# Attention ahead of two gated MLPs: each head's scores and values as matmuls on their own part of the TensorE array

## The chip, the cores and the metric

The kernel runs on one core of one Trainium2 chip. The metric is device time in microseconds from the first to the last instruction of one execution. The shown time of the kernel before is the median of three runs; the profile is one more execution, recorded by the hardware profiler.

## The reference

Shapes: q, k, v are (2, 8, 768, 64); the output is (2, 768, 512). All inputs are float32.

```python
# attention: a band of +-15 keys, and one key for each block of 32 (max of k, mean of v)
k_sum = k.reshape(B, H, nb, 32, D).max(axis=3)
v_sum = v.reshape(B, H, nb, 32, D).mean(axis=3)
scores_l = np.where(|i - j| < 16, scale * q @ k.T, -1e9)
scores_s = scale * q @ k_sum.T + log(32)
a = softmax(concat[scores_l, scores_s])
x = (a @ concat[v, v_sum])            # -> (B, S, H * D)
# first gated MLP: a causal depthwise convolution with 5 taps makes the gate
x = sigmoid(conv(x, conv_w)) * (x @ w_val) @ w_out
# second: gating through a matmul over the sequence
h = relu(x @ w_in); u, v = split(h)
v_n = layernorm(v)
out = (u * (w_spatial @ v_n + b)) @ w_out2
```

## The kernel before

**Stages.** The attention stage takes 54 steps and fills the first third of the execution. Behind it come `x @ w_val` with the convolution, the product of `w_out` and `w_in` ("fused"), the `u` and `v` products, the product with `w_spatial` and the output product. Those behind the attention are written as split fp32r matmuls, all in `product` (L858).

**Tiling of the attention.** The 16 (batch, head) pairs are taken two heads at a time: 8 pairs p of heads, six tiles t of 128 rows each, so 48 steps i. The two heads of a pair lie in partitions 0 to 63 and 64 to 127 (their 64 channels each). A tile of 128 rows is two groups of 64 rows; a group sees 96 near keys and 24 block keys, 120 in all.

- `turn_k`, `turn_q` (L739): TensorE transposes of k and q into PSUM, two for a piece of 256 rows; three pieces of k and three of q for each pair of heads, one piece a step. k of all 128 partitions is copied to `k_win` in one piece (VectorE, L1340).
- q is copied to `qT` in two pieces. `qT` is a block-diagonal array: for each group 128 columns, of which the first 64 hold head 0 in partitions 0 to 63 (ScalarE, L1022) and the last 64 hold head 1 in partitions 64 to 127 (VectorE, L1351). The other two quarters are zeros, written once at the start (L1401).
- `scores` (L774): one matmul for each of the two groups, with the 128x128 block of `qT` as the stationary operand and 128x120 of `k_win` moving. The zeros keep the heads apart: out come 64 rows of head 0 and 64 of head 1.
- `mask_scores` (VectorE, L1313), `exponentials` (ScalarE, L1034, two a step), `normalise` (VectorE, L1333).
- `turn_probs` (L788): two TensorE transposes a step; `take_probsT` (ScalarE, L1048) copies both out of PSUM.
- `values` (L803): one matmul for each group, 120x128 of `v_win` (both heads' channels) stationary and 120x128 of `probsT` (both heads' rows) moving. All four combinations of head and head come out; only the two diagonal blocks of 64x64 are used.
- `take_x` copies the attention output to `xT` once for every two steps: head 0's blocks on ScalarE (L1054), head 1's on ScalarE as well (L1057), or on VectorE (L1358) for the 7 of 24 that `x_on_dve` names.
- `means` (L815) sums v over blocks, three matmuls for each pair of heads.

**What sets the order.** Everything is written out by hand: each engine has its own loop over the steps and waits on semaphores. TensorE's step i is: scores(i), one turned piece of the next pair, turn_probs(i-5), values(i-6). ScalarE's is: take_probsT(i-5), turned_q, exponentials(i), take_x on even steps. SyncE issues all loads in one queue, two pairs ahead for k and q, one for v.

## Time and profile before

| | |
|---|---|
| median of 3 runs | 296.59 us (296.08 to 296.78) |
| the profiled execution | 294.5 us, of which 292.8 us are the span of the trace |
| granted TensorE clock | 1.00 (2.4 GHz) over the whole span |
| TensorE matmul busy | 282.2 us, 96%, 1828 matmuls |
| VectorE busy | 226.1 us, 77% |
| ScalarE busy | 181.4 us, 62% |
| GpSimd busy | 91.7 us, 31% |
| DMA engines, q1 | 35.0% of 16 engines' span |

The stages follow each other, so these shares are averages over stages with different limits. Matmuls are pipelined: one that is busy for 0.27 us lets the next one start 0.11 us later, so what a stretch of TensorE costs is read from starts, not from busy time. An fp32 matmul that is written once shows as two records, a transpose as one.

### The profile page before, as it was taken

To read this page: it belongs to the slowest core of one execution; us is meant where nothing else is said; L and a number is where in the kernel's file an instruction comes from. 1 tells how busy PE (TensorE), PEld (TensorE's weight loads), DVE (VectorE), ACT (ScalarE), POOL (GpSimd) and SP (SyncE) were. 2 spreads that over 40 slices of the span, in tenths; PEclk is the share of its full clock that TensorE was granted. 3 is DMA by queue.
4 is the path that set the end of the run, shared out by engine and by line. 5 is a ranking of instruction groups with operands and counts; after the bars stand their busy time and mean duration, and the time that the engine had idled before them with its cause. 6 is when DMAs were issued, how large, how long until landed. Compare 5 with 4: busy or idle time off the path is not lost.

```text
span 292.8 us, 5673 instructions
## 1 busy us (share of the span) xinstructions
PE 282.2 (96%) x1828; PEld 264.8 (90%) x1828; DVE 226.1 (77%) x632; ACT 181.4 (62%) x517; POOL 91.7 (31%) x111
## 2 busy tenths in 40 slices
PE   7879999999999999899999999999999999999996
PEld 7769999999989998798899988998889999999996
DVE  6798999999788989993202676895867989898952
ACT  3579999999998567454354455625258342644632
POOL 6425778898433898325000000000007000000000
PEclk9999999999999999999999999999999999999999
DMA  7998999999520443000040000000021000001324
GB/s 159 218 264 175 247 196 231 221 184 216 150 73 2 158 120 119 0 0 3 0 154 10 0 0 2 0 0 2 0 72 73 2 1 0 2 0 56 140 77 161
DMA packets 52474, 25.54 MB, mean 87 GB/s; under 512 B 44618, under 2 KB 48222, under 8 KB 52446
## 3 DMA queue, kind: packets, MB, share of 16 engines
q1 hardware_dynamic: 52446, 25.18, 35.0%
q8 instruction: 15, 0.25, 0.4%
q14 instruction: 13, 0.11, 0.1%
HBM read 22.03 MB, written 3.15 MB: 86 GB/s over the span
## 4 chain that ended last, share of the span: by engine, by line
PE 67%; ACT 17%; DVE 7%; issue 5%; POOL 2%; DMA 1%; DVEq 0%; ACTq 0%; POOLq 0%
PE psum L858 57%; ACT probs L1034 8%; DVE psum L1387 4%; PE psum L774 2%; ACT qT L1022 2%; PE psum L803 2%; ACT xT L1054 2%; PE psum L739 2%; PE psum L834 1%; ACT probsT L1048 1%; PE psum L788 1%; PE psum L935 1%; ACT xT L1057 1%; DMA raw<-in_moe_w_in_dram 1%; DVE work L1452 1%
## 5 line engine op out<-in xcount | busy, mean ns | idle before, releaser
L1034 ACT ACTIVATE probs<-neg_s,neg_max 128x120 f32<-128x120 f32 x96 | 36.8, 387 | 0.3 <-DVE neg_max L1313 0.3
L686 POOL TENSOR_TENSOR vn_lo<-vn_all,vn_hi 128x768 fp32r<-128x768 f32 x3 | 5.8, 1958 | 83.0 <-ACT vn_hi L1155 83.0
L803 PE MATMUL psum<-probsT,v_win 120*128 120x128 f32 x192 | 29.9, 278 | 0.0
L774 PE MATMUL psum<-k_win,qT 128*128 128x120 f32 x192 | 29.0, 274 | 0.7 <-DVE qT L1351 0.7
L1387 DVE SCALAR_TENSOR_TENSOR psum<-xT,conv_c,psum 128x384 f32<-128x384 f32 x48 | 26.0, 615 | 1.2 <-ACT psum L1076 1.2
L1313 DVE CUSTOM_DVE_ANT_0 neg_s<-psum,mask 128x120 f32<-128x120 f32 x96 | 24.5, 276 | 2.6 <-PE psum L774 2.2
L774 PEld LDWEIGHTS psum<-k_win,qT 128*128 128x128 f32 x192 | 25.2, 192 | 1.2 <-issue 0.9
L803 PEld LDWEIGHTS psum<-probsT,v_win 120*128 120x128 f32 x192 | 25.2, 191 | 0.4
L788 PE MATMUL psum<-ident,probs 128*120 128x128 f32 x96 | 19.1, 281 | 2.8 <-ACT probsT L1048 2.2
L1048 ACT ACTIVATE probsT<-psum 120x256 f32<-120x256 f32 x48 | 18.1, 376 | 3.4 <-PE psum L788 3.0
L1333 DVE TENSOR_TENSOR probs<-probs,psum 128x240 f32<-128x240 f32 x48 | 19.0, 400 | 1.0
L686 POOL TENSOR_TENSOR g_lo<-work,g_hi 128x384 fp32r<-128x384 f32 x16 | 15.9, 1019 | 11.8 <-ACT g_hi L1124 11.8
L1034 ACT ACTIVATION_READ_ACCUMULATOR probs<-neg_s,neg_max 128x1 f32 x96 | 18.6, 194 | 0.0
L788 PEld LDWEIGHTS psum<-ident,probs 128*120 128x120 f32 x96 | 11.1, 137 | 6.6 <-ACT probsT L1048 5.7
L1198 ACT ACTIVATE u<-psum 128x384 f32<-128x384 f32 x16 | 7.8, 487 | 14.0 <-PE psum L858 13.7
L1469 DVE TENSOR_TENSOR wsp_lo<-wsp_all,wsp_hi 128x1152 fp32r<-128x1152 f32 x3 | 4.0, 1355 | 14.5 <-ACT wsp_hi L1142 14.5
L686 POOL TENSOR_TENSOR x_lo<-xT,x_hi 128x768 fp32r<-128x768 f32 x8 | 14.6, 1829 | 0.6
L667 POOL COPY v_win<-v_mean 24x1536 f32<-24x1536 f32 x8 | 11.7, 1462 | 8.6 <-ACT v_mean L1064 7.5
L858 PE MATMUL psum<-g_hi,wu_hi 128*128 128x384 f32 x64 | 14.4, 346 | 0.0
L1076 ACT ACTIVATE psum<-xT,conv_c 128x384 f32<-128x384 f32 x16 | 8.7, 573 | 9.1 <-DVE gate L1387 9.1
L1526 DVE BATCH_NORM_STATS2 stats<-work 128x6 f32<-128x512 f32 x12 | 8.3, 691 | 7.7 <-ACT work L1209 7.7
L858 PE MATMUL psum<-x_hi,wval_hi 128*128 128x384 f32 x64 | 14.1, 341 | 0.0
(183 smaller groups left out, 829.4 us busy)
## 6 DMA issues: line engine op xcount, KB each, us to landing
v_win<-in_v_dram SPq DMA_DIRECT2D x16, 240.0 KB, 3.8
k_nat<-in_k_dram SPq DMA_DIRECT2D x16, 192.0 KB, 4.9
v_nat<-in_v_dram SPq DMA_DIRECT2D x8, 384.0 KB, 3.8
q_nat<-in_q_dram SPq DMA_DIRECT2D x14, 192.0 KB, 4.4
raw<-in_moe_w_spatial_dram SPq DMA_DIRECT2D x6, 384.0 KB, 3.1
raw<-in_moe_w_in_dram SPq DMA_DIRECT2D x8, 256.0 KB, 3.1
out_dram<-rows SPq DMA_DIRECT2D x12, 128.0 KB, 1.7
out_dram<-rows SPq DMA_DIRECT2D x6, 256.0 KB, 2.0
```

Source lines behind the costliest of these rows:

```text
L667: nc.gpsimd.tensor_copy(v_win[NEAR:KEYS, p % 2, :, :], src).then_inc(means_spread, 1)
L686: nc.gpsimd.tensor_tensor(dst_lo, src, dst_hi.bitcast(F32), ALU.subtract).then_inc(lo_sem, 1)
L774: ins = nc.tensor.matmul(bank_s(i)[:, g, :], qT[:, s, 2 * t + g, :], k_win[:, s, 2 * t + g, :], start=True, stop=True)
L788: ins = nc.tensor.transpose(bank_t[:, g, :], probs[:, i % RING, g, :], ident[:, :])
L803: ins = nc.tensor.matmul(bank_x(i)[:, i % 2 * 2 + g, :], v_win[0:KEYS, s, 2 * t + g, :], probsT[0:KEYS, i % 2, g, :], start=True, stop=True)
L858: ins = nc.tensor.matmul(o, lhs[a][c], rhs[b][c], start=(fresh and part == 0 and c == 0), stop=(part == 2 and c == n - 1), skip_group_chec ...
L1034: ins = nc.scalar.activation(probs[:, i % RING, g, :], neg_s[:, i % 3, g, :], ACT.Exp, bias=neg_max[:, i % 4, g:g + 1], scale=-1.0, accum_ ...
L1048: nc.scalar.activation(probsT[0:KEYS, i % 2, :, :], bank_t, ACT.Copy).then_inc(probsT_ready, 1)
L1076: nc.scalar.activation(psum[:, 4 + half, 0:HALF], x_of(p, half * HALF, HALF), ACT.Copy, scale=conv_c[:, (TAPS - 1) * C + c:(TAPS - 1) * C ...
L1313: nc.vector.tensor_tensor_reduce(out=neg_s[:, i % 3, g, :], in0=bank_s(i)[:, g, :], in1=mask[:, e, :], scale=-(float(D) ** -0.5), scalar=B ...
L1333: nc.vector.tensor_tensor(a, a, r, ALU.mult).then_inc(probs_ready, 1)
L1387: nc.vector.scalar_tensor_tensor(out=o, in0=x, scalar=w, in1=acc, op0=ALU.mult, op1=ALU.add).then_inc(conv_step, 1)
```

## The change

`scores` and `values` are cut by head. For each group and each head h there is one matmul of its own, on partitions and columns of its head alone:

- scores: stationary 64x64 of `qT` (64 channels of head h, 64 rows), moving 64x120 of `k_win`, output to PSUM partitions 64h to 64h+63. Head 0 uses rows 0 to 63 and columns 0 to 63 of the array, head 1 rows 64 to 127 and columns 64 to 127.
- values: stationary 120x64 of `v_win` (the head's channels), moving 120x64 of `probsT` (the head's rows), output to PSUM partitions 64h to 64h+63.

`qT` has 64 columns for each group in place of 128 and no zeros; its two memsets go. One ScalarE copy of 128x256 takes a piece of q; VectorE's is gone. `bank_x` has 64 columns for each group, and one ScalarE copy of 128x256 takes two steps' output; ScalarE's second copy and VectorE's seven are gone, and so is `x_on_dve`. Three semaphores stand where there were six.

```diff
-            qT = sb("qT", [P, 2, GROUPS, P], F32, att)
+            qT = sb("qT", [P, 2, GROUPS, GROUP], F32, att)
...
         def bank_x(i):
-            return psum[:, 6 + (i // 2) % 2, :].rearrange("p (g n) -> p g n", n=P)
-
-        def x_on_dve(j):
-            return j % 3 == 1 and 2 * j < STEPS - 4
+            return psum[:, 6 + (i // 2) % 2, 0:2 * P].rearrange("p (g n) -> p g n", n=GROUP)
...
             def scores(i):
...
                 if t % 2 == 0:
-                    pe.wait_ge(qA_ready, PIECES * p + t // 2 + 1)
-                    pe.wait_ge(qB_ready, PIECES * p + t // 2 + 1)
+                    pe.wait_ge(qT_ready, PIECES * p + t // 2 + 1)
...
                 for g in range(2):
-                    ins = nc.tensor.matmul(bank_s(i)[:, g, :], qT[:, s, 2 * t + g, :], k_win[:, s, 2 * t + g, :],
-                                           start=True, stop=True)
+                    for h in range(2):
+                        d, rows_of = slice(h * D, (h + 1) * D), slice(h * GROUP, (h + 1) * GROUP)
+                        ins = nc.tensor.matmul(bank_s(i)[rows_of, g, :], qT[d, s, 2 * t + g, :],
+                                               k_win[d, s, 2 * t + g, :], start=True, stop=True, skip_group_check=True)
...
             def values(i):
...
                 for g in range(2):
-                    ins = nc.tensor.matmul(bank_x(i)[:, i % 2 * 2 + g, :], v_win[0:KEYS, s, 2 * t + g, :],
-                                           probsT[0:KEYS, i % 2, g, :], start=True, stop=True)
+                    for h in range(2):
+                        d, rows_of = slice(h * D, (h + 1) * D), slice(h * GROUP, (h + 1) * GROUP)
+                        ins = nc.tensor.matmul(bank_x(i)[d, i % 2 * 2 + g, :], v_win[0:KEYS, s, 2 * t + g, d],
+                                               probsT[0:KEYS, i % 2, g, rows_of], start=True, stop=True,
+                                               skip_group_check=True)
...
         def _(act):
             def turned_q(p, piece):
...
-                nc.scalar.activation(qT[0:D, p % 2, n * piece:n * (piece + 1), 0:GROUP],
-                                     by_group(bank_qk(PIECES + piece)[0:D]), ACT.Copy).then_inc(qA_ready, 1)
+                nc.scalar.activation(qT[:, p % 2, n * piece:n * (piece + 1), :],
+                                     by_group(bank_qk(PIECES + piece)), ACT.Copy).then_inc(qT_ready, 1)
...
             def take_x(j):
...
-                nc.scalar.activation(by_group(x_of(p, r * P, 2 * P)[0:D]), bank_x(2 * j)[0:D, :, 0:GROUP],
-                                     ACT.Copy).then_inc(xA_ready, 1)
-                if not x_on_dve(j):
-                    nc.scalar.activation(by_group(x_of(p, r * P, 2 * P)[D:P]), bank_x(2 * j)[D:P, :, GROUP:P],
-                                         ACT.Copy).then_inc(xB_ready, 1)
+                nc.scalar.activation(by_group(x_of(p, r * P, 2 * P)), bank_x(2 * j), ACT.Copy).then_inc(x_ready, 1)
...
         def _(dve):
...
-            def turned_q(p, piece):
...
-            def take_x(j):
...
-            for s in range(2):
-                nc.vector.memset(qT[:, s, :, :], 0.0).then_inc(q_zeros, 1)
```

TensorE in the middle of the attention stage, a step and the start of the next, before. The numbers are output partitions x moving columns, and x2 counts matmuls as written (each fp32 matmul of L774 and L803 is two records in the trace):

```order
L739 MATMUL psum<-ident,k_nat 128x128 x2
L788 MATMUL psum<-ident,probs 120x128 x2
L803 MATMUL psum<-probsT,v_win 128x128 x2
L774 MATMUL psum<-k_win,qT 128x120 x2
L739 MATMUL psum<-ident,k_nat 128x128 x2
```

The same place after; the lines have other numbers there (L727, L775, L792, L761):

```order
L727 MATMUL psum<-ident,k_nat 128x128 x2
L775 MATMUL psum<-ident,probs 120x128 x2
L792 MATMUL psum<-probsT,v_win 64x64 x4
L761 MATMUL psum<-k_win,qT 64x120 x4
L727 MATMUL psum<-ident,k_nat 128x128 x2
```

The order of the kinds is the same. Values and scores are four matmuls each in place of two, and they alone don't use the whole array.

ScalarE over three steps in the middle of the stage, before:

```order
L1054 ACTIVATE xT<-psum 64x256
L1057 ACTIVATE xT<-psum 64x256
L1048 ACTIVATE probsT<-psum 120x256
L1022 ACTIVATE qT<-psum 64x4x64
L1034 ACTIVATE probs,sums<-neg_s,neg_max 128x120 x2
L1048 ACTIVATE probsT<-psum 120x256
L1022 ACTIVATE qT<-psum 64x4x64
L1034 ACTIVATE probs,sums<-neg_s,neg_max 128x120 x2
L1054 ACTIVATE xT<-psum 64x256
```

And after:

```order
L1040 ACTIVATE xT<-psum 128x256
L1034 ACTIVATE probsT<-psum 120x256
L1008 ACTIVATE qT<-psum 128x256
L1020 ACTIVATE probs,sums<-neg_s,neg_max 128x120 x2
L1034 ACTIVATE probsT<-psum 120x256
L1008 ACTIVATE qT<-psum 128x256
L1020 ACTIVATE probs,sums<-neg_s,neg_max 128x120 x2
L1040 ACTIVATE xT<-psum 128x256
```

The second copy of the attention output is gone, and the copies of q and of the output write 128 partitions in place of 64.

## Rows read from the trace of the kernel before

**Rows 1.** The page: busy time, share of the span, instructions of each engine.

```profile
PE 282.2 (96%) x1828; PEld 264.8 (90%) x1828; DVE 226.1 (77%) x632; ACT 181.4 (62%) x517; POOL 91.7 (31%) x111
```

**Rows 2.** Busy time by stretch; the last three columns: clock, DMA share, GB/s.

```profile
core 0: us, PE busy (x) PEld busy (x) DVE busy (x) ACT busy (x) POOL busy (x), PEclk, DMA share, GB/s
...
49.50:58.80 9.30, 9.09 (x79) 8.60 (x79) 8.98 (x48) 9.15 (x40) 7.88 (x10) 1.00 0.92 210
...
120.00:162.00 42.00, 42.00 (x231) 38.52 (x231) 19.12 (x33) 20.00 (x40) 7.96 (x8) 1.00 0.09 29
```

**Rows 3.** Chain that ended last, parts in the middle of the attention stage.

```profile
52.55 0.75 ACT probs L1034 x4
...
53.33 0.13 issue
53.47 0.37 ACT qT L1022
53.83 0.76 ACT probs L1034 x4
54.59 0.23 ACT xT L1054
```

**Rows 4.** ScalarE in order of time: start, length, line, operation.

```profile
51.11 0.36 ACT L1054 ACTIVATE xT<-psum 64x256 f32<-64x256 f32 x1
51.50 0.38 ACT L1057 ACTIVATE xT<-psum 64x256 f32<-64x256 f32 x1
51.90 0.38 ACT L1048 ACTIVATE probsT<-psum 120x256 f32<-120x256 f32 x1
```

**Rows 5.** TensorE in order of time, one step and the next.

```profile
49.49 0.43 PE L788 MATMUL psum<-ident,probs 128*120 128x128 f32 x2 [0.17 <-ACT probsT L1048]
49.76 0.62 PE L803 MATMUL psum<-probsT,v_win 120*128 120x128 f32 x4
50.22 0.60 PE L774 MATMUL psum<-k_win,qT 128*128 128x120 f32 x4
50.66 0.38 PE L739 MATMUL psum<-ident,q_nat 128*128 128x128 f32 x2
50.88 0.38 PE L788 MATMUL psum<-ident,probs 128*120 128x128 f32 x2
51.10 0.61 PE L803 MATMUL psum<-probsT,v_win 120*128 120x128 f32 x4
51.54 0.60 PE L774 MATMUL psum<-k_win,qT 128*128 128x120 f32 x4
```

**Rows 6.** TensorE in order of time: block means, then first values of four pairs.

```profile
53.73 0.82 PE L815 MATMUL psum<-v_nat,sel 128*120 128x128 f32 x6
54.38 0.38 PE L788 MATMUL psum<-ident,probs 128*120 128x128 f32 x2
...
18.11 0.61 PE L803 MATMUL psum<-probsT,v_win 120*128 120x128 f32 x4
...
46.66 0.68 PE L803 MATMUL psum<-probsT,v_win 120*128 120x128 f32 x4
55.92 0.67 PE L803 MATMUL psum<-probsT,v_win 120*128 120x128 f32 x4
...
84.82 0.68 PE L803 MATMUL psum<-probsT,v_win 120*128 120x128 f32 x4
```

**Rows 7.** The page's groups: busy us, mean ns of one.

```profile
L774 PE MATMUL psum<-k_win,qT 128*128 128x120 f32 x192 | 29.0, 274 | 0.7 <-DVE qT L1351 0.7
```

**Rows 8.** TensorE later: matmuls of 384 columns, then of 256.

```profile
102.40 0.85 PE L858 MATMUL psum<-x_hi,wval_hi 128*128 128x384 f32 x4
103.09 0.85 PE L858 MATMUL psum<-x_hi,wval_lo 128*128 128x384 f32 x4
...
262.39 0.40 PE L858 MATMUL psum<-wout_hi,g_hi 128*128 128x256 f32 x2
262.62 0.40 PE L858 MATMUL psum<-wout_hi,g_lo 128*128 128x256 f32 x2
```

**Rows 9.** TensorE in the last six steps of the attention.

```profile
87.42 0.38 PE L788 MATMUL psum<-ident,probs 128*120 128x128 f32 x2
87.64 0.61 PE L803 MATMUL psum<-probsT,v_win 120*128 120x128 f32 x4
88.00 0.96 PE L858 MATMUL psum<-x_hi,wval_hi 128*128 128x384 f32 x4
88.80 0.38 PE L788 MATMUL psum<-ident,probs 128*120 128x128 f32 x2
```

**Rows 10.** ScalarE and VectorE groups by form; last, one line's durations min/median/max.

```profile
L1048 ACT ACTIVATE probsT<-psum 120x256 f32<-120x256 f32 x48 | 18.1, 376 | 3.4 <-PE psum L788 3.0
L1022 ACT ACTIVATE qT<-psum 64x256 f32<-64x256 f32 x24 | 8.8, 371 | 2.6 <-PE psum L739 2.4
...
L1351 DVE COPY qT<-psum 64x256 f32<-64x256 f32 x24 | 10.2, 427 | 1.0 <-PE psum L739 0.3
...
L1057 ACT ACTIVATE xT<-psum x17: 378/378/382, 23.6 to 93.0; 64x256 f32<-64x256 f32 x17
```

**Rows 11.** Chain that ended last, at the start of the attention stage.

```profile
15.71 0.43 DVE qT L1351
...
17.08 0.44 DVE qT L1351
```

**Rows 12.** SyncE's queue in order of time; then v's small loads, last number us to landing.

```profile
44.70 3.00 SPq L520 DMA_DIRECT2D k_nat<-in_k_dram  x2
...
51.97 0.42 SPq L534 DMA_DIRECT2D v_win<-in_v_dram  x1
...
54.61 1.74 SPq L520 DMA_DIRECT2D k_nat<-in_k_dram  x2
...
v_win<-in_v_dram SPq DMA_DIRECT2D x32, 20.0 KB, 3.0
```

**Rows 13.** First TensorE rows of the execution.

```profile
1.58 3.46 PE L834 MATMUL psum<-ident 128*128 128x128 f32 x15 [1.58 <-POOL ident L690]
4.84 1.73 PE L739 MATMUL psum<-ident,k_nat 128*128 128x128 f32 x6
6.40 1.04 PE L834 MATMUL psum<-ident 128*128 128x128 f32 x8
7.28 0.38 PE L739 MATMUL psum<-ident,q_nat 128*128 128x128 f32 x2
```

More of the change, by code:

```diff
@@ L203, in attention_gated_mlp @@
         conv_turned = sem("conv_turned")
-        qA_ready = sem("qA_ready")
-        qB_ready = sem("qB_ready")
+        qT_ready = sem("qT_ready")
         kT_ready = sem("kT_ready")
@@ L219, in attention_gated_mlp @@
         x_summed = sem("x_summed")
-        xA_ready = sem("xA_ready")
-        xB_ready = sem("xB_ready")
-        xD_ready = sem("xD_ready")
+        x_ready = sem("x_ready")
         x_hi_ready = sem("x_hi_ready")
@@ L305, in bank_x @@
         def bank_x(i):
-            return psum[:, 6 + (i // 2) % 2, :].rearrange("p (g n) -> p g n", n=P)
-        def x_on_dve(j):
-            return j % 3 == 1 and 2 * j < STEPS - 4
+            return psum[:, 6 + (i // 2) % 2, 0:2 * P].rearrange("p (g n) -> p g n", n=GROUP)
         def wait_x(eng, tiles):
-            n = tiles // 2
-            eng.wait_ge(xA_ready, n)
-            on_dve = sum(x_on_dve(j) for j in range(n))
-            eng.wait_ge(xB_ready, n - on_dve)
-            if on_dve:
-                eng.wait_ge(xD_ready, on_dve)
+            eng.wait_ge(x_ready, tiles // 2)
         def rows(w, n, cols=slice(None)):
@@ L745, in turn_k @@
                 if piece < 2 and p >= 1:
-                    pe.wait_ge(qA_ready, PIECES * (p - 1) + 2 + piece)
-                    pe.wait_ge(qB_ready, PIECES * (p - 1) + 2 + piece)
+                    pe.wait_ge(qT_ready, PIECES * (p - 1) + 2 + piece)
                 elif piece == 2:
@@ L756, in turn_q @@
                 else:
-                    pe.wait_ge(qA_ready, PIECES * p + 1)
-                    pe.wait_ge(qB_ready, PIECES * p + 1)
+                    pe.wait_ge(qT_ready, PIECES * p + 1)
                 turn(q_nat, p, piece, q_loaded, q_turned)
@@ L823, in turn_wout @@
                 else:
-                    pe.wait_ge(qA_ready, PIECES * (PAIRS - 1) + 2 + c)
-                    pe.wait_ge(qB_ready, PIECES * (PAIRS - 1) + 2 + c)
+                    pe.wait_ge(qT_ready, PIECES * (PAIRS - 1) + 2 + c)
                 for n in range(C):
@@ L1013, in turned_q @@
             def turned_q(p, piece):
-                if piece == 0:
-                    if p < 2:
-                        act.wait_ge(q_zeros, p + 1)
-                    else:
-                        act.wait_ge(scores_ready, T * (p - 1))
+                if piece == 0 and p >= 2:
+                    act.wait_ge(scores_ready, T * (p - 1))
                 act.wait_ge(q_turned, PIECES * p + piece + 1)
                 n = PIECE // GROUP
-                nc.scalar.activation(qT[0:D, p % 2, n * piece:n * (piece + 1), 0:GROUP],
-                                     by_group(bank_qk(PIECES + piece)[0:D]), ACT.Copy).then_inc(qA_ready, 1)
+                nc.scalar.activation(qT[:, p % 2, n * piece:n * (piece + 1), :],
+                                     by_group(bank_qk(PIECES + piece)), ACT.Copy).then_inc(qT_ready, 1)
             def first_k(piece):
@@ L1408, in _ @@
                     mask_scores(i, g)
-            for piece in range(1, PIECES):
-                turned_q(0, piece)
             dve.wait_ge(eps_set, 1)
@@ L1431, in _ @@
                     invert_sums((i - 3) // 2)
-                if i >= 8 and i % 2 == 0 and x_on_dve((i - 8) // 2):
-                    take_x((i - 8) // 2)
                 if p == PAIRS - 1 and t - 1 in WOUT_AT:
```

17 lines of the change are left out of this document (removed).

## The prediction

> **What bounds the kernel now.** I read the page first: TensorE is busy 96% of the span [rows 1], but the stages have different limits, so the stretches by stage come next. In the attention stage four engines are all close to full: in the 9.30 us of one pair of heads TensorE is busy 9.09, VectorE 8.98, ScalarE 9.15 [rows 2]. Behind it, from 120 us on, TensorE alone is full. The change touches only the attention stage, so the question is which of the engines there ends last. The chain of waits answers: in the middle of the stage it runs on ScalarE for microseconds on end, exponentials, copy of q, exponentials, copy of the output, with "issue" gaps of some 0.1 us [rows 3]. In order of time ScalarE starts one instruction after the other without a hole: from the first copy of the attention output to the second 0.39 us, from there to probsT 0.40 [rows 4]. TensorE has holes: 0.17 us ahead of the transposes of the probabilities, until ScalarE has copied probsT [rows 5].
>
> What TensorE needs for a pair of heads is read from starts. Four records of scores, 50.22 to 50.66, are 0.44 us; two transposes of q, 50.66 to 50.88, are 0.22; two of the probabilities 0.22; four records of values, 51.10 to 51.54, are 0.44 [rows 5]. That is 1.32 a step, 7.92 for six, and with the block means, 53.73 to 54.38, 8.57 us [rows 6]. The stage gives it 9.53: the first values of pair 0 start at 18.11, those of pair 7 at 84.82, seven pairs in 66.7 us, the undisturbed ones 9.3 apart [rows 6]. **So ScalarE bounds the stage with TensorE 0.7 us a pair behind it.** Whatever TensorE gets over 0.7 us a pair is paid for in full.
>
> **The change, part by part.**
>
> *ScalarE's second copy of the output.* 17 of them, 378 ns each [rows 10], 0.39 from start to start [rows 4]. They lie on the chain's engine: 2 or so a pair, 0.78 us. The copies that stay write 128 partitions in place of 64; the copy of probsT has 120 partitions and takes 376 ns, that of q has 64 and takes 371 [rows 10], so width in partitions is free. ScalarE alone would go at 9.30 - 0.78 = 8.5 us a pair. But then TensorE's 8.57 is late next: even if the matmuls cost nothing more, a pair falls to 8.6, a gain of 0.7.
>
> *VectorE's copies.* 24 of q, 427 ns [rows 10], and 7 of the output go. In the middle of the stage VectorE isn't on the chain, so they are worth nothing there. At the start two of them are: 0.43 and 0.44 us, at 15.71 and 17.08 [rows 11]. ScalarE's copy of the same piece still has to be made, and it comes behind exponentials; I take 0.5 of the 0.87. The two memsets of `qT` end before the first k has been copied, so their end saves nothing. No engine gets a new wait: TensorE's waits for two copies become waits for one.
>
> *The matmuls.* Scores: 4 matmuls of 64x64 by 120 columns a step in place of 2 of 128x128 by 120. Values: 4 of 120x64 by 64 in place of 2 of 120x128 by 128. In records it is 8 and 8 in place of 4 and 4. The trace has no matmul on a part of the array, so three costs are unknown and have to be bounded.
>
> (a) Values. Half the columns, twice the records. From 384 columns to 256 a record goes from 0.69/4 = 0.173 to 0.23/2 = 0.117 us [rows 8], in proportion to the columns; by that 64 columns take half of 0.11, and eight records 0.44, as before. No row has fewer than 120 columns in a stream, so the other end is no discount at all: 8 x 0.11 = 0.88. I take the proportional end, since two rows show it.
>
> (b) Scores. The columns stay 120, the records double. If head 1's matmul, on the other half of rows and columns, runs beside head 0's, a step's scores stay at 0.44; if they run one after another it is 0.88. The trace shows neither. I take 0.44.
>
> (c) Changes between the whole array and parts of it. A step now goes scores (parts of 64x64), transposes (whole), values (parts of 128x64), scores: three changes a step, 18 a pair, which the order shows. If the array has to run empty before it is divided otherwise, each costs two things. A matmul lasts 274 ns [rows 7] and the next starts 0.11 after it, so 0.16 us of it is overlap that is lost. And the start from empty costs something more: after the 0.17 us hole the two transposes and the next start take 49.76 - 49.49 = 0.27 in place of 0.22 [rows 5], so 0.05. Bounds: nothing, or 0.05 (only the restart), up to 0.21. I take 0.13, halfway between 0.05 and 0.21: weights loaded ahead may hide a part.
>
> What the hardware does here no row shows. The Trainium skill ("TensorEngine Tiling (Array Packing)", section "Key Properties") says that changing the tiling mode drains TensorE; it gives no price. The same section says that different tiles work in parallel, which is what (b) takes.
>
> **The sum.** TensorE needs 8.57 + 18 x 0.13 = 10.9 us a pair. It becomes the bound; ScalarE's 8.5 and VectorE's, with fewer copies, hide below it. Seven pairs take 76.4 in place of 66.7: +9.7. The last six steps, from 84.5 to 91.5, have no scores but matmuls of `x @ w_val` between values and transposes, and TensorE goes from one to the next without a hole [rows 9]: two changes a step, 12 x 0.13 = +1.6. The start: -0.5. Together +10.8. What follows the attention (GpSimd's split of x, the convolution) is released by its last copies and moves along as it is. Profiled execution 294.5 + 10.8 = 305.3; the median of the runs stands 2.1 above the profiled one, so **307 us** is the forecast.
>
> **Rivals.**
>
> *Only one of (b) and (c), the other one.* Heads one after another and no price for changes: 8.57 + 6 x 0.44 = 11.2 a pair, +11.7, -0.5: 308. The same number by another cause; I count it with the forecast, as I do (c) at its upper end, 8.57 + 18 x 0.21 = 12.35, +19.7 + 2.5 - 0.5: 318.
>
> *Everything at once.* Serial heads and changes at 0.13: 13.6 us a pair, +28 + 1.6 - 0.5: 326. Or a record costs 0.11 however small it is: 126 records and more, 8.57 + 48 x 0.11 = 13.9, +30 + 2.6 in the last steps: 329. For it: no record in this trace starts less than some 0.11 behind the one before, transposes of 128 columns and fp32 matmuls of 120 alike [rows 5]. Against it: [rows 8].
>
> *The array takes it for nothing (the side of a gain).* Heads run side by side and changes cost under 0.04. Then a pair takes 8.6: 7 x 0.7 = -4.9; the last steps lose two copies that are on the chain, -0.8; the start -0.5: 294.5 - 6.2 + 2.1 = 290. It decides at 18 changes x 0.04 = 0.7 us. Something takes part of it back: SyncE issues one pair's loads in 9.9 us, 44.70 to 54.61, without a wait for another engine, and v's last piece is issued at 51.97, lands some 3.0 us later, and is used at 55.92 [rows 6, 12]. About 1 us is spare, and from pair 4 on loads would hold the stage: 293. For it: TensorE's holes, the shorter ScalarE list. Against it: it needs three unknown costs to be zero. The Trainium skill (same page, "Theoretical Speedup") promises up to twice the rate for dimensions of 64; by that scores and values would fall to 0.22 each and ScalarE's 8.5 would be all that is left, which with the loads is this rival again.
>
> *Changes cost the restart alone, 0.05.* 9.5 us a pair, as long as now: 296, no change.
>
> *The clock falls.* The granted clock is 1.00 in every stretch [rows 2]. The first 15 identity transposes are 3.26/15 = 0.217 apart, the later 8 are 0.11 [rows 13]: that is what the lower level of 1.2 GHz costs. If an array used in parts counted as idle, a pair would take 17 us: 350. TensorE would still have work nearly all the time, so I give it little.
>
> **How the numbers follow.** Forecast (one of the two costs, 300 to 318): 0.40. Everything at once (325 to 330): 0.20. For nothing (290 to 293.5): 0.28. Restart alone (about 296): 0.07. Clock: 0.05. The predicted time is the forecast's, 307. The range goes from 290 to 328: it leaves out the clock, the upper part of the second case and the lowest of the third, less than 2 in 10. Most of the chance lies on the slower side, whose own range is 299 to 329. A measurement of this kernel can tell about 0.2%, 0.6 us, from no change. Faster 0.29, same 0.05, slower 0.66.
>
> **What would show it.** In the trace after: ScalarE has holes before probsT and before the copy of q, and the chain goes over to TensorE's scores, values and transposes. If (c) is right, holes stand in TensorE's order of time at each change of kind, of 0.1 to 0.2 us, and none between values' or scores' own records. If (b) fails, eight score records take 0.88 us. If (a) fails, eight value records do. If the change is free, ScalarE stays without a hole, a pair takes 8.6 us, and the first wait of a matmul for v's load appears about pair 4. The forecast would be wrong first by (c): it is the term with the widest bounds and counts 18 times a pair.

## The result and the profile after

The median after is 300.13 us (297.74 to 300.64, 13 runs), beside 295.13 us before (293.74 to 298.21, 13 runs, those shown above among them). The ratio is 1.0148, interval 1.0123 to 1.0173: 1.5% slower. The forecast, 307 beside 296.59, was 3.5% slower. The sign and the bound came out, the size is less than half. Where executions of one kernel lie over 1.5% apart, ratios go by the fast ones; this bears on one kernel below. The profiled execution took 298.75 us, span 296.9, which is 4.1 more than the span before.

The page after: TensorE's busy row, then the chain that ended last by engine, then three groups (busy us, mean ns | idle before them and its releaser).

```profile
PE 289.4 (97%) x2212; PEld 256.9 (87%) x2212; DVE 211.7 (71%) x599; ACT 175.9 (59%) x500; POOL 91.7 (31%) x111
...
PE 93%; SPq 4%; DMA 2%; issue 0%; DVE 0%
...
L761 PE MATMUL psum<-k_win,qT 64*64 64x120 f32 x384 | 30.3, 278 | 0.6 <-ACT qT L1008 0.6
L1034 ACT ACTIVATE probsT<-psum 120x256 f32<-120x256 f32 x48 | 18.3, 381 | 14.4 <-PE psum L775 13.1
...
L792 PE MATMUL psum<-probsT,v_win 120*64 120x64 f32 x384 | 21.9, 236 | 0.0
```

ScalarE's copies of probsT now wait 14.4 us in all for the transposes, where the same group stood at 3.4 in [rows 10], and behind the first loads nothing but TensorE is left on the chain, where ScalarE ran for microseconds on end in [rows 3]. So TensorE has become the bound. One hole of ScalarE in order of time, which answers to the gapless [rows 4]:

```profile
54.06 0.38 ACT L1034 ACTIVATE probsT<-psum 120x256 f32<-120x256 f32 x1 [0.40 <-PE psum L775]
```

TensorE in order of time, one step and the next (this answers to [rows 5]), then the first values of the next pair of heads and the last values of all:

```profile
49.38 0.45 PE L792 MATMUL psum<-probsT,v_win 120*64 120x64 f32 x8
49.76 0.63 PE L761 MATMUL psum<-k_win,qT 64*64 64x120 f32 x8
50.32 0.44 PE L727 MATMUL psum<-ident,k_nat 128*128 128x128 f32 x2
50.59 0.38 PE L775 MATMUL psum<-ident,probs 128*120 128x128 f32 x2
50.90 0.45 PE L792 MATMUL psum<-probsT,v_win 120*64 120x64 f32 x8
...
60.72 0.45 PE L792 MATMUL psum<-probsT,v_win 120*64 120x64 f32 x8
...
97.23 0.45 PE L792 MATMUL psum<-probsT,v_win 120*64 120x64 f32 x8
```

A step lasts 50.90 - 49.38 = 1.52 us without a wait, and a pair of heads 60.72 - 50.90 = 9.82, where it was 9.3 before and the forecast said 10.9.

There is a second effect, at the start of the stage. TensorE waits 2.66 us for a piece of k, and the rows that come 1.5 us later are stretched:

```profile
18.75 0.41 PE L727 MATMUL psum<-ident,k_nat 128*128 128x128 f32 x2 [2.66 <-DMA k_nat<-in_k_dram]
...
20.25 0.68 PE L727 MATMUL psum<-ident,k_nat 128*128 128x128 f32 x2
...
21.91 1.06 PE L761 MATMUL psum<-k_win,qT 64*64 64x120 f32 x8
```

Busy time by stretch, with the columns of [rows 2]:

```profile
21.60:30.90 9.30, 9.30 (x110) 7.29 (x107) 5.52 (x31) 6.68 (x29) 4.34 (x6) 0.89 0.94 214
49.50:58.80 9.30, 9.30 (x124) 7.09 (x125) 7.08 (x42) 8.60 (x37) 7.36 (x10) 1.00 0.94 212
```

Eight records of scores from 21.91 last until 22.90, 0.99 us, where they are 0.56 later, and the stretch from 21.6 has a granted clock of 0.89: for some 3.4 us the clock was at 1.2 in place of 2.4 GHz. The mean granted clock of the 13 runs tells how often: one run had 1.000 and took 297.74 us, four had 0.994 (298.75 to 299.82; the profiled one with its single drop is among them), eight had 0.988 or 0.989 (299.86 to 300.64). So most runs after lose about twice what the profiled one does.

**Where the time went in the profiled execution.** Differences of starts, after less before:

| | before | after | difference |
|---|---|---|---|
| first values of pair 0 | 18.11 | 19.31 | +1.2 |
| from there to the first values of pair 7 | 66.7 | 70.6 | +3.9 |
| from there to the last values | 84.82 to 91.53 | 89.90 to 97.23 | +0.6 |
| the rest | | | -1.6 |
| span | 292.8 | 296.9 | +4.1 |

Of the 1.6 us that come back, one row of before names 1.05. Behind the attention TensorE had one wait, for a split of a weight on VectorE. It is absent after; the kernel with two copies, below, tells which copy it hung on. The row of before:

```profile
119.80 1.19 PE L858 MATMUL psum<-win_u_hi,woutT_hi 128*128 128x512 f32 x4 [1.05 <-DVE wu_lo L1461]
```

### The profile page after: what moved, and what is told of

It is laid out like the page before. It is cut to its first block, busy times and chain, and to the rows that moved or that the text cites. A ratio compares the mean times of both kernels' runs of the same rounds, so it can differ in the third digit from the quotient of the medians.

```text
span 296.9 us, 6320 instructions
## 1 busy us (share of the span) xinstructions
PE 289.4 (97%) x2212; PEld 256.9 (87%) x2212; DVE 211.7 (71%) x599; ACT 175.9 (59%) x500; POOL 91.7 (31%) x111
## 4 chain that ended last, share of the span: by engine, by line
PE 93%; SPq 4%; DMA 2%; issue 0%; DVE 0%
PE psum L847 67%; PE psum L761 8%; PE psum L792 6%; PE psum L727 5%; PE psum L775 4%; DMA k_nat<-in_k_dram 2%; PE psum L805 2%; PE psum L924 1%; SPq L508 1%; SPq L521 1%; PE psum L816 1%; SPq L547 1%; SPq L520 0%; SPq L529 0%; SPq L522 0%
## 5 line engine op out<-in xcount | busy, mean ns | idle before, releaser
L761 PE MATMUL psum<-k_win,qT 64*64 64x120 f32 x384 | 30.3, 278 | 0.6 <-ACT qT L1008 0.6
L1034 ACT ACTIVATE probsT<-psum 120x256 f32<-120x256 f32 x48 | 18.3, 381 | 14.4 <-PE psum L775 13.1
L761 PEld LDWEIGHTS psum<-k_win,qT 64*64 64x64 f32 x384 | 19.5, 134 | 4.4 <-issue 1.3
L792 PEld LDWEIGHTS psum<-probsT,v_win 120*64 120x64 f32 x384 | 15.3, 138 | 8.4 <-issue 8.4
L792 PE MATMUL psum<-probsT,v_win 120*64 120x64 f32 x384 | 21.9, 236 | 0.0
L775 PE MATMUL psum<-ident,probs 128*120 128x128 f32 x96 | 18.7, 277 | 0.0
L847 PE MATMUL psum<-g_hi,wu_hi 128*128 128x384 f32 x64 | 14.4, 346 | 0.0
L727 PE MATMUL psum<-ident,k_nat 128*128 128x128 f32 x48 | 11.2, 328 | 2.8 <-DMA k_nat<-in_k_dram 2.7
L847 PE MATMUL psum<-x_hi,wval_lo 128*128 128x384 f32 x64 | 13.9, 338 | 0.0
```

The costliest lines, as they stand in the source:

```text
L727: ins = nc.tensor.transpose(bank_qk(piece + PIECES * (src is q_nat))[:, a * P:(a + 1) * P], src[:, p % n, 2 * piece + a, :], ident[:, :])
L761: ins = nc.tensor.matmul(bank_s(i)[rows_of, g, :], qT[d, s, 2 * t + g, :], k_win[d, s, 2 * t + g, :], start=True, stop=True, skip_group_ch ...
L775: ins = nc.tensor.transpose(bank_t[:, g, :], probs[:, i % RING, g, :], ident[:, :])
L792: ins = nc.tensor.matmul(bank_x(i)[d, i % 2 * 2 + g, :], v_win[0:KEYS, s, 2 * t + g, d], probsT[0:KEYS, i % 2, g, rows_of], start=True, st ...
L847: ins = nc.tensor.matmul(o, lhs[a][c], rhs[b][c], start=(fresh and part == 0 and c == 0), stop=(part == 2 and c == n - 1), skip_group_chec ...
L1034: nc.scalar.activation(probsT[0:KEYS, i % 2, :, :], bank_t, ACT.Copy).then_inc(probsT_ready, 1)
```

## The experiments

The theory behind the forecast (A): a change between whole array and parts costs TensorE 0.13 us or so, and the heads run side by side. Rivals: the time comes from the heads or the records themselves; from the one copy in place of two; from the clock. Each kernel is the kernel before or after with the edit shown. Pairs are measured from first values to first values.

**One half of the change alone.** The first has only `values` cut by head (and the dense copy of its output), the second only `scores` (and the dense q).

```diff
# values alone, from the kernel before
-                    ins = nc.tensor.matmul(bank_x(i)[:, i % 2 * 2 + g, :], v_win[0:KEYS, s, 2 * t + g, :],
-                                           probsT[0:KEYS, i % 2, g, :], start=True, stop=True)
+                    for h in range(2):
+                        d, rows_of = slice(h * D, (h + 1) * D), slice(h * GROUP, (h + 1) * GROUP)
+                        ins = nc.tensor.matmul(bank_x(i)[d, i % 2 * 2 + g, :], v_win[0:KEYS, s, 2 * t + g, d],
+                                               probsT[0:KEYS, i % 2, g, rows_of], start=True, stop=True, ...)
```

> Only the values are cut by head, with the dense attention output and its one copy; scores stay whole on the block-diagonal q with its two copies. Theory A (each change between the whole array and parts of it costs TensorE 0.15 us, both heads' parts run side by side, everything else is streaming): TensorE 6 x (0.44 + 0.44 + 0.23 + 2 x 0.15) + 0.65 = 9.1 us a pair, just above ScalarE's 8.5: some 0.2 to 0.4 a pair less than before, ratio to before 0.990 to 0.997. Theory B (no price for changes, but 0.03 us for each record of a small matmul): 8.7 a pair, ratio 0.98. Theory C (the stage is held by loads and the first clock drop, not by TensorE): as the changed kernel, 1.015.

> Only the scores are cut by head, with dense q and its one copy; values stay whole, with ScalarE's and VectorE's second copies of the output. Theory A: TensorE 6 x (0.41 + 0.44 + 0.44 + 2 x 0.15) + 0.65 = 10.2 us a pair, slower than the full change's 9.8: ratio to before 1.02 to 1.03. Theory B: 9.8 a pair, ratio 1.01. Theory C: 1.015 or less.

Values alone: 293.85 us beside 294.98, ratio 0.9952 (0.9921 to 0.9983): faster than either kernel. A pair takes 9.375 us (28.44 to 65.94 for four). Scores alone: 302.4, ratio 1.0232 (1.0189 to 1.0276), a pair 10.21 (31.70 to 72.53 for four). Both are within 0.3 us a pair of what A said. The gain with values alone isn't in the pairs, which took 9.3 before: its last values start at 91.83, beside 91.53. It lies behind the attention, where the wait of 1.05 us for VectorE is absent from its trace too, though TensorE hardly comes later there. With scores alone, where the output keeps its two copies, the wait of 1.05 stands. TensorE in order of time, first values alone, then scores alone:

```profile
47.19 0.45 PE L797 MATMUL psum<-probsT,v_win 120*64 120x64 f32 x8
47.58 0.70 PE L766 MATMUL psum<-k_win,qT 128*128 128x120 f32 x4
48.12 0.38 PE L731 MATMUL psum<-ident,k_nat 128*128 128x128 f32 x2
48.34 0.38 PE L780 MATMUL psum<-ident,probs 128*120 128x128 f32 x2
48.65 0.45 PE L797 MATMUL psum<-probsT,v_win 120*64 120x64 f32 x8
```

```profile
52.12 0.61 PE L800 MATMUL psum<-probsT,v_win 120*128 120x128 f32 x4
52.66 0.63 PE L771 MATMUL psum<-k_win,qT 64*64 64x120 f32 x8
53.22 0.44 PE L737 MATMUL psum<-ident,k_nat 128*128 128x128 f32 x2
...
53.71 0.61 PE L800 MATMUL psum<-probsT,v_win 120*128 120x128 f32 x4
```

Whole scores take 0.44 us up to the next start between matmuls of the whole array [rows 5] and 0.54 behind the values' parts. Whole values take 0.54 ahead of the scores' parts, where they took 0.44. The extra stands at the changes and nowhere else. With values alone the step is 1.46, with scores alone 1.59. Cutting the scores gains next to nothing and pays for two changes; cutting the values gains 0.2 and pays for two.

**More changes.** A matmul of 64x64 by 8 columns is put between the two transposes of each of the 48 turns of k and q, where it makes two changes more; in a second kernel the same matmul stands ahead of a step's scores, where it makes none.

```diff
# more changes, from the kernel after (in the turns of k and q)
+                    if a == 0:
+                        nc.tensor.matmul(psum[0:D, 4 + ... % 2, 2 * P:2 * P + 8],
+                                         ident[0:D, 0:D], ident[0:D, 0:8], start=True, stop=True, ...)
# no more changes (in scores)
+                nc.tensor.matmul(psum[0:D, i % 2, 2 * P:2 * P + 8], ident[0:D, 0:D], ident[0:D, 0:8], ...)
```

> The changed kernel with one more small matmul (64x64 stationary, 8 columns, result not used) in each of the 48 turns of k or q, between the two whole-array transposes: two more changes of the array's division each, 96 in all. Theory A: 48 x 2 x 0.15 = +14 us on the changed kernel, ratio to before 1.06. Theory B: 96 small records x 0.03 = +3 us, ratio 1.025.

> The changed kernel with the same small matmul 48 times, but ahead of a step's first scores matmul, which is on the same part of the array: no more changes. Theory A: only its own streaming and loading, 48 x 0.05 = +2.5 us at most, ratio to before 1.015 to 1.025. Theory B: as the one between the transposes.

More changes: 345.0, 311.02, 327.94 and 311.31 us. The ratio, 1.0524 (1.0455 to 1.0592), is that of the two at 311: 11 us on the kernel after, where A said 14. Their mean granted clock is 1.000, though, and beside the one run of the kernel after that had this too, 297.74, it is 13.4 us, 0.14 for each of 96 changes with the small matmuls' own cost in it. No more changes: 305.2, ratio 1.0316 (1.0268 to 1.0364), 5 us on the kernel after, which is more than expected. Three rows of the first kernel, from the profiled execution of 345.0 us:

```profile
52.02 1.07 PE L765 MATMUL psum<-k_win,qT 64*64 64x120 f32 x8
...
90.94 0.45 PE L796 MATMUL psum<-probsT,v_win 120*64 120x64 f32 x8
...
92.83 0.45 PE L796 MATMUL psum<-probsT,v_win 120*64 120x64 f32 x8
```

The first row is 1.07 us long, where 0.63 is usual: up to 89 us that execution ran at half rate. Behind that it ran at the usual one, and a step with two changes more takes 92.83 - 90.94 = 1.89 us. The second kernel's step takes 1.64 (52.54 to 54.18), so the small matmul costs 0.11 where nothing changes. Since it costs something by itself, a whole-run difference alone doesn't give the price of a change, and the pair was repeated in one execution: twelve more changes in pair 4 of heads alone, and the matmul ahead of the scores in pair 5 alone.

```diff
+                    if a == 0 and p == 4:
+                        nc.tensor.matmul(...)   # between the two transposes
...
+                if p == 5:
+                    nc.tensor.matmul(...)       # ahead of the scores
```

> The changed kernel with the extra small matmul in the six turns made during one pair of heads (between two whole-array transposes: 12 more changes), and ahead of the scores of six steps of another pair (no more changes, beside the same part), the rest as it was. Theory A: in the trace the first of these pairs takes 9.82 + 12 x 0.15 = 11.6 us, the second at most 9.82 + 6 x 0.11 = 10.5, the others 9.82. Theory B: both the same, 10.2.

One execution of 302.68 us, span 301.0. The stretch with twelve more changes takes 11.97 us (40.78 to 52.75, values to values), the other 10.47 (62.56 to 73.03), where 11.6 and at most 10.5 were expected. TensorE in order of time, scores and the next scores in one pair, then the small matmul and the next one in the other:

```profile
48.70 0.63 PE L768 MATMUL psum<-k_win,qT 64*64 64x120 f32 x8
49.26 0.33 PE L727 MATMUL psum<-ident,q_nat 128*128 128x128 f32 x1
49.52 0.28 PE L730 MATMUL psum<-ident 64*64 64x8 f32 x2
...
50.59 0.63 PE L768 MATMUL psum<-k_win,qT 64*64 64x120 f32 x8
```

```profile
62.94 0.22 PE L763 MATMUL psum<-ident 64*64 64x8 f32 x1
62.96 0.31 PE L768 MATMUL psum<-k_win,qT 64*64 64x120 f32 x1
63.02 0.20 PE L763 MATMUL psum<-ident 64*64 64x8 f32 x1
...
64.58 0.22 PE L763 MATMUL psum<-ident 64*64 64x8 f32 x1
```

1.89 us a step with two changes more, 1.64 with the matmul alone, 1.52 with neither. A change costs (1.89 - 1.64)/2 = 0.13 if the matmul costs 0.11 in both places, and (1.89 - 1.52)/2 = 0.18 if it costs nothing between the transposes. The rows give the first of the two changes by itself: from the transpose at 49.26 to the small matmul at 49.52 it is 0.26 us, where one transpose starts 0.11 behind another, so 0.15. It is a single run, so its time is not compared.

**Is it the copy?** The attention output copied in two halves, both on ScalarE.

```diff
-                nc.scalar.activation(by_group(x_of(p, r * P, 2 * P)), bank_x(2 * j), ACT.Copy).then_inc(x_ready, 1)
+                for d in (slice(0, D), slice(D, P)):
+                    nc.scalar.activation(by_group(x_of(p, r * P, 2 * P)[d]), bank_x(2 * j)[d], ACT.Copy).then_inc(x_ready, 1)
```

> The changed kernel with the dense attention output copied in two halves of 64 partitions again, both on ScalarE: 24 copies more, 0.39 us each from start to start. ScalarE would need 8.5 + 3 x 0.39 = 9.7 us a pair, TensorE's 9.8 still ends last. Theory A: no change on the changed kernel, at most +1 us: ratio to before 1.015 to 1.018. If the one copy was worth something after all, up to +9 us, 1.045.

301.28 us, ratio 1.022 (1.018 to 1.0259): above the kernel after by 1.2 us by the medians, by 2.1 by the two ratios. In the middle a pair still takes 9.82 (39.59 to 69.03 for three), so there the copy lies beside TensorE. The profiled execution has a granted clock of 1.00 throughout and a span of 297.5 us, 1.9 more than that of the kernel after with its clock held (295.6, next experiment). Of this 1.05 stand by the last values, where ScalarE also splits weights and TensorE waits for it, and the rest behind the attention:

```profile
89.12 0.43 PE L775 MATMUL psum<-ident,probs 128*120 128x128 f32 x2 [0.60 <-ACT probsT L1034]
...
124.62 1.19 PE L847 MATMUL psum<-win_u_hi,woutT_hi 128*128 128x512 f32 x4 [0.74 <-DVE wu_lo L1416]
```

The second row is the wait of 1.05 us of before again. VectorE's list is that of the kernel after, so VectorE's missing copies are not what removed it. It stands in the three kernels with a second copy of the output on ScalarE (before 1.05, scores alone 1.05, this one 0.74) and in none of the others. So the saved copies, worth 0.78 us a pair on the chain of before, are worth about 2 us in all once TensorE bounds.

**Is it the clock?** 24 identity transposes ahead of the piece of k that TensorE waits for.

```diff
+                if i == T:
+                    for _ in range(24):
+                        nc.tensor.transpose(psum[:, 7, 3 * P:4 * P], ident[:, :], ident[:, :])
```

> The changed kernel with 24 identity transposes (2.6 us, into a bank that nothing reads then) ahead of the first turn of k of pair 2, where TensorE waited 2.7 us for a load and its granted clock was halved 1.6 us after the wait, for 3.4 us. If that wait is why the clock falls, it stays at 1.00 and the stage is some 1.7 us shorter: ratio to before 1.009. If it falls for another reason (parts of the array counting less), it falls anyway and the ratio stays at 1.015.

```profile
15.77 2.84 PE L893 MATMUL psum<-ident 128*128 128x128 f32 x24
18.76 0.41 PE L727 MATMUL psum<-ident,k_nat 128*128 128x128 f32 x2 [0.15 <-DMA k_nat<-in_k_dram]
...
20.26 0.44 PE L727 MATMUL psum<-ident,k_nat 128*128 128x128 f32 x2
```

297.75 us, ratio 1.0084 (1.0052 to 1.0116). The load lands when it did (18.76 beside 18.75), the row at 20.26 has its usual 0.44 in place of 0.68, and the granted clock of all six runs is 1.00 (0.999 once). 297.75 is also what the one run of the kernel after without a drop took, 297.74. So the clock, set off by a wait of TensorE for a load, makes 1.9 us (by the two ratios) to 2.4 (by the medians) of the loss of about 5. The rest, some 2.5 us by the ratio, is a balance: by its trace +1.2 at the start, +2.4 for the seven pairs, +0.6 in the last steps and -1.4 behind them.

**Fewer changes, by blocks of two steps.** Values of two steps, scores of two steps, and then the transposes of both; probsT has four buffers. Three changes for two steps in place of six (with the whole change), two in place of four (with values alone).

```diff
+                if i >= 8 and i % 2 == 0:
+                    values(i - 8)
+                    values(i - 7)
-                if 2 <= i < STEPS:
+                if 2 <= i < STEPS and i % 2 == 0:
                     scores(i)
+                    scores(i + 1)
...
-                if 6 <= i:
-                    values(i - 6)
```

> The changed kernel with TensorE's order in blocks of two steps: four values, four more values, eight scores, then the two steps' transposes each; probsT has four buffers in place of two. Three changes of the array's division for two steps in place of six; every matmul is the same. Theory A: TensorE 6 x (0.41 + 0.44 + 0.23 + 1.5 x 0.15) + 0.65 = 8.5 us a pair in place of 9.8, level with ScalarE's 8.5; 7 pairs save up to 9 us, less what loads and latencies take back: ratio to before 0.97 to 0.99. Theory B (a price for each small record): as the changed kernel or a little above, 1.015.

> Values by head, scores whole (as the values-only kernel), in the same blocks of two steps: two changes for two steps. Theory A with the 0.17 us a change of the values-only trace: TensorE 6 x (0.44 + 0.44 + 0.23 + 0.17) + 0.65 = 8.3 us a pair, ScalarE's 8.5 bounds: ratio to before 0.97 to 0.985. If loads hold the stage, as the prediction's third case has it, both block kernels stop near 9 a pair, ratio 0.985.

299.41 us, ratio 1.0147 (1.0113 to 1.0181), and 296.32, ratio 1.0039 (1.0011 to 1.0067): neither gains. The first kernel's TensorE, one block and the start of the next:

```profile
49.21 0.69 PE L792 MATMUL psum<-probsT,v_win 120*64 120x64 f32 x16
49.83 1.04 PE L761 MATMUL psum<-k_win,qT 64*64 64x120 f32 x16
50.80 0.44 PE L727 MATMUL psum<-ident,k_nat 128*128 128x128 f32 x2
...
51.93 0.43 PE L775 MATMUL psum<-ident,probs 128*120 128x128 f32 x2 [0.26 <-ACT probsT L1038]
52.29 0.39 PE L792 MATMUL psum<-probsT,v_win 120*64 120x64 f32 x6
```

Two steps take 3.08 us, because the second step's turned probabilities have to wait until ScalarE has copied the first's out of the one bank. But the rows hold what no kernel so far showed: 16 records of values take 0.62 us up to the next start and 16 of scores 0.97, where 8 take 0.38 and 0.56. So eight further records cost 0.24 and 0.41, with no change among them. In the second kernel a pair takes 9.82 us (27.91 to 37.73), more than the 9.375 of values alone in the plain order; TensorE waits 4.2 us in all for ScalarE's copies of probsT.

**The same with a bank for each of the two.** The reciprocals move to SBUF, which frees the bank, and the waits that guard the banks follow; otherwise as above.

```diff
-        bank_t = psum[0:KEYS, 2, 0:2 * P].rearrange("p (g n) -> p g n", n=P)
+        def bank_t(i):
+            return psum[0:KEYS, 2 + i % 2, 0:2 * P].rearrange("p (g n) -> p g n", n=P)
...
-            return psum[:, 3, i % 4 * 2:i % 4 * 2 + 2]
+            return recips[:, i % 4 * 2:i % 4 * 2 + 2]
```

> The block kernel with a PSUM bank of its own for each of the two steps' turned probabilities (the reciprocals move from that bank to SBUF). In the block kernel TensorE stood 0.42 us every two steps, because the second step's transposes of the probabilities had to wait for ScalarE's copy out of the one bank. If that wait is all that ate the gain, two steps take 3.08 - 0.47 = 2.6 us, a pair 8.5, level with ScalarE: ratio to before 0.975 to 0.99. If fewer changes bring nothing in themselves, it stays at 1.015.

> The same for the values-only block kernel: 3.05 - 0.47 = 2.6 us for two steps, TensorE 8.4 a pair, ScalarE's 8.5 bounds. Ratio to before 0.97 to 0.985; where loads of v come late, 0.985 to 0.99.

301.28 us, ratio 1.024 (1.0206 to 1.0274), and 302.05, ratio 1.0239 (1.0202 to 1.0277): both slower. The first:

```profile
46.84 0.63 PE L763 MATMUL psum<-k_win,qT 64*64 64x120 f32 x8 [0.75 <-DVE neg_max L1302]
...
49.59 0.69 PE L795 MATMUL psum<-probsT,v_win 120*64 120x64 f32 x16
...
52.20 0.51 PE L795 MATMUL psum<-probsT,v_win 120*64 120x64 f32 x10
```

Where nothing is waited for, two steps take 2.61 us, as A has it. But once a pair the second scores of a block wait 0.75 us for VectorE's mask of the scores two steps earlier, the block means wait 0.26 for ScalarE, and a pair takes 10.06 (49.59 to 59.65). The chain goes over ScalarE's exponentials and VectorE's masks and normalising from 43.87 to 46.84. With values alone the waits are of the same kind (0.67 for the mask once a pair), and a pair takes 10.55 (36.89 to 47.44). That the scores come in twos, and give VectorE and ScalarE their work in lumps, is the likely reason; the next kernel, which leaves the scores alone, bears it out. So fewer changes do save time on TensorE, and a new wait eats the whole gain.

**Values in twos, scores every step.** The values-only kernel, and every odd step takes the values of two steps; the scores stay where they were.

```diff
-                if 6 <= i:
-                    values(i - 6)
+                if 6 <= i and i % 2 == 1:
+                    values(i - 7)
+                    values(i - 6)
```

> The values by head alone (scores, q and their copy as before), and the values of two steps together on every odd step, behind the scores; the scores come every step, as in the kernel before, and the turned probs have four buffers. So there are two changes between whole array and parts for two steps in place of four, and the scores of two steps do not have to be ready together, which ate the gain where the order went in blocks of two steps. Theory A (each change costs about 0.15 us, the parts run side by side): two steps lose 2 x 0.15 to 0.17 = 0.3 us against the kernel with the values alone by head, TensorE comes to 6 x (0.44 + 0.44 + 0.23 + 0.17) + 0.65 = 8.3 us a pair of heads, ScalarE's 8.5 would bound it, and the ratio to the kernel before is 0.975 to 0.99. Rival: a wait that the new order brings eats it, as in the block kernels, and the ratio is 0.995 or more, with a wait of TensorE for ScalarE or VectorE in every pair of heads.

291.77 us beside 294.61, ratio 0.9881 (0.9851 to 0.9911): 1.2% faster than before and 2.6% faster than the kernel after. One block, and the waits of two pairs:

```profile
49.60 0.41 PE L731 MATMUL psum<-ident,q_nat 128*128 128x128 f32 x2 [0.68 <-DMA q_nat<-in_q_dram]
...
50.16 0.69 PE L797 MATMUL psum<-probsT,v_win 120*64 120x64 f32 x16
50.77 0.70 PE L766 MATMUL psum<-k_win,qT 128*128 128x120 f32 x4
51.31 0.38 PE L731 MATMUL psum<-ident,q_nat 128*128 128x128 f32 x2
...
51.75 0.60 PE L766 MATMUL psum<-k_win,qT 128*128 128x120 f32 x4
...
69.54 0.41 PE L731 MATMUL psum<-ident,q_nat 128*128 128x128 f32 x2 [1.56 <-DMA q_nat<-in_q_dram]
```

Scores behind values have 0.54 (50.77 to 51.31), scores behind transposes 0.44 (51.75 to 52.19): a change costs only where there is one. Two steps without block means take 29.15 to 31.75, 2.60. That is 8.45 a pair for TensorE, near A's 8.3. A pair takes 8.8 us (29.15 to 37.95 to 46.73), with the chain on VectorE and ScalarE from 27.9 to 37.6, until loads take over: 9.35, 9.70 and 10.6 for the next three, with waits for q of 0.68, 1.02 and 1.56 us. SyncE issues q every 9.45 to 10.2 us (35.09, 44.54, 54.11, 64.32). That is the limit that the rival "for nothing" named. Of the 2.6 us that the span is shorter than before, the last values account for 1.3 (90.27 beside 91.53), and the wait of 1.05 behind the attention is absent here as well.

## Why the prediction was right in its sign and wrong in its size

**The bound.** Right. TensorE had 0.7 us a pair to spare, took more than that, and ScalarE's list, shorter by a copy, went off the chain.

**(c) The changes.** Right, with some luck: 0.13 was taken as the middle of two bounds. The kernel after gives it by parts: values 0.38 up to the next start less 0.24 of their own, 0.14; scores 0.56 - 0.41 = 0.15; the four transposes 0.58 less 0.44, 0.14. Two changes cost 1.46 - 0.44 - 0.44 - 0.24 = 0.34 with values alone and 1.59 - 0.44 - 0.44 - 0.41 = 0.30 with scores alone, and a change in the middle of the transposes 0.13 to 0.18. The Trainium skill ("TensorEngine Tiling (Array Packing)", "Key Properties") says that changing the mode drains the engine; the holes at each change agree with that, and about 0.15 us is what this kernel pays. The prediction hoped that "weights loaded ahead may hide a part". The first weight load of a step's scores, before and after:

```profile
51.43 0.53 PEld L774 LDWEIGHTS psum<-k_win,qT 128*128 128x128 f32 x4
...
51.28 0.40 PEld L761 LDWEIGHTS psum<-k_win,qT 64*64 64x64 f32 x8
```

Before, it starts 0.11 us ahead of its matmul, which is at 51.54 [rows 5], while values are still running. After, it starts with its matmul, at 51.28, and so it is at the other two changes of the step (50.90 and 51.84). No weights are loaded ahead across a change, so nothing of that kind hides it.

**(b) The scores' heads side by side.** Right: 0.41 for eight records of 120 columns, where 0.44 was taken and 0.88 would be one after another. Taken singly, the records start in twos, the two heads' 0.007 us apart, and one such two follows the other after 0.10 us (after 0.06 for the values' 64 columns).

**(a) The values.** This is the step that failed. The prediction said: half the columns, "by that 64 columns take half of 0.11, and eight records 0.44, as before". The columns did count in proportion. But it multiplied by eight records in a row, and the values' two heads run side by side too, since they use different columns of the array. Eight records take 0.24. The condition that (b) had allowed the scores, "on the other half of rows and columns", is not needed: the values' parts share the rows and differ in columns alone. Six steps times 0.20 is 1.2 us a pair, 8.4 in seven pairs.

The sum with the measured terms: 8.57 - 6 x 0.20 - 6 x 0.03 + 18 x 0.147 = 9.84, beside 9.82 measured. From 10.9 that is -1.1 a pair, -7.6 over seven. Of these, -8.4 are the values, -1.3 the scores, +2.1 the changes. With the clock held, the seven pairs take 69.1 us (19.32 to 88.41) in place of the forecast's 76.4: -7.3. Everything else is smaller and partly goes the other way.

**Start: -0.5.** Wrong sign. VectorE's two copies did go, but what came late behind them was a load of k: by the chain it took from 13.02 to 18.62, and the first values came 1.2 us later than before. The prediction took a stall away and didn't look for the load behind it. In the trace before the same load had landed by about 17.5 (its second part issued at 13.3, 4.2 us at most to landing), just ahead of the 17.64 at which TensorE's wait for VectorE ended, so without the stall little could be gained even there. Why it landed later after is open. It goes with the scores: in the seven profiled executions that have them by head and show the wait (other than the one with the clock held and the one at half rate) TensorE waited 2.25 to 3.09 us for this load, until 18.32 to 19.67; in the four with values alone by head it waited at most 1.63.

**The clock.** It was a rival with the wrong mechanism: the prediction feared that parts of the array count as idle. The granted clock stays at 1.00 through stretches full of parts (49.5 to 58.8). It fell after a wait for a load, for a few microseconds, and cost 1.5 us in the profiled execution (first values of pair 7 at 89.90, beside 88.41 with the clock held). The kernel before has it in fewer runs: 18 of the 56 beside the experiments showed 0.993 or 0.994, and of the last 11 the five with 0.994 took 295.88 to 296.12, the six with 1.000 took 294.48 to 294.61. One thing stays open for this rival: the kernel with most changes had up to 89 us at half rate, and whether its changes have to do with that wasn't tried.

**The last six steps: +1.6.** Its two changes a step are there, but the values' gain of 0.2 stands against them, and the measured difference from the first values of pair 7 to the last values is 0.6. **What follows moves along as it is:** wrong by 1.6 us, of which 1.05 is the wait for VectorE. It was in the trace before, and the prediction gave ScalarE's second copy, on which the runs show it to hang, no worth behind the attention.

Terms together, for the profiled execution: +10.8 forecast; -7.3 for the seven pairs, +1.7 for the start, +1.5 for the clock, -1.0 for the last steps, -1.6 behind: +4.1, as the span has it. The 2.1 us that the forecast added for the median over the profiled execution came from three runs; over 13 runs they are 0.6.

**The rivals.** "Changes cost the restart alone" gave 9.5 us a pair, nearer to 9.82 than the forecast's 10.9, by two errors that nearly cancel: 0.05 a change where it is 0.15, and values at 0.44 where they are 0.24. "For nothing" used the statement of the Trainium skill (same page, "Theoretical Speedup") of up to twice the rate for dimensions of 64. The rows show it for the values, 0.24 beside 0.44, but not for the scores, which streamed 120 columns through the whole array in 0.44 before and stream the same in 0.41. A product whose zeros fill the array's other half already costs no more than its halves side by side; one whose moving operand holds both heads costs twice.

## What to carry to other kernels

Ask of each matmul that is cut into parts of the array whether the parts stream fewer columns: where only zeros go (the scores), time stays and the changes of division are all that is added; where half the moving columns go (the values), the time halves. Then count the changes between whole array and parts, at 0.15 us each, and put matmuls of one division next to each other without making the other engines' work come in lumps. When TensorE gets faster, look next at the loads, and at any wait of some microseconds, which can cost clock besides itself.

## What the runs showed of the hardware

- A change between whole array (128x128) and parts (64x64 or 120x64), or between the two kinds of parts (values to scores), costs TensorE about 0.15 us each time (0.13 to 0.18), and weights are not loaded ahead across it.
- Two heads' matmuls on parts that differ in rows and columns, or in columns alone with different moving operands, run side by side, in fp32: eight records of 120 columns 0.41 us, of 64 columns 0.24. The two heads' scores go to one PSUM bank, to different partitions of it.
- A 64x64 matmul of 8 columns ahead of the scores costs 0.11 us, though it changes no division. It doesn't break the pairing of the heads: a record of scores starts at 62.96, between the small matmul's two at 62.94 and 63.02, and the other seven follow from 63.08. One head's part has two records more. Why they take 0.11 us with so few columns wasn't tried.
- After a wait of 2.66 us the granted clock went to its lower level about 1.5 us later, for some 3.4 us. Five other profiled executions show such a fall, with waits of 2.25, 2.30, 2.82, 2.99 and 3.09 us for the same load, and it came 0.1 to 0.4 us behind the wait, or within it (2.99, for 6.8 us). With 2.28 us of wait (the kernel with two copies) it didn't come in the profiled execution, so the length of the wait alone doesn't tell.
- One execution of the kernel with most changes (345 us) ran at half rate from its first matmuls to 89 us, and at full rate behind, with no fall in the clock row. That row is 1.00 over the first microseconds of the other kernels too, where the identity transposes are 0.217 apart in place of 0.11 [rows 13]. So the row doesn't show the low rate at the start, and here that rate lasted longer; why is open.
